# Handing the experts' last rows from ScalarE to VectorE and SyncE, and splitting the last quarter of the output weight in later tiles

## The reference

```python
# 1: q, k, v (2, 8, 768, 64), state (64 x 64) for each head
for t in range(S):
    state = gamma * state + k[t] v[t]^T
    y[t] = scale * q[t] state
# 2: x (1536, 512), 8 experts, w1 (8, 512, 1024), w2 (8, 1024, 512), capacity 384
e = argmax(x @ w_gate); gate = softmax(x @ w_gate)[e]
out[i] = gate * (relu(x[i] @ w1[e]) @ w2[e])      # the first 384 tokens of each expert
# 3: x (1536, 512), w_in (512, 2048), w_out (2048, 512)
h = x @ w_in
P = a0 + a1*h + a2*h^2 + a3*h^3
Q = 1 + |b0|*|h| + |b1|*h^2
out = (P / (Q + 1e-6)) @ w_out
```

## Time and profile before

| | |
|---|---|
| runs | 549.85 us median of 3 (548.81 to 549.91) |
| the profiled execution | 548.83 us, span of the trace 547.0 us |
| granted TensorE clock | 1.00 in all of stage 3 |
| busy, share of the span | TensorE 98%, VectorE 74%, ScalarE 59%, GpSimd 13% |
| stage 2 ends, TensorE's first matmul of stage 3 | 274.2 us |

### The profile page before, as it was taken

The page is one execution under the profiler, slowest core; times in us unless marked ns, Lnnn a source line. Parts: engine busy times, 40 slices in busy tenths (PEclk is TensorE's granted clock), DMA queues, the critical chain, the costliest instruction groups (busy, mean ns, idle before and its releaser), DMA issues.

```text
span 547.0 us, 8985 instructions
## 1 busy us (share of the span) xinstructions
PE 536.8 (98%) x3405; PEld 461.6 (84%) x3405; DVE 404.5 (74%) x737; ACT 320.8 (59%) x484; POOL 73.4 (13%) x71
## 2 busy tenths in 40 slices
PE   8999999999999999999989999999999999999997
PEld 6888889898998989999877878888888888888885
DVE  4567777654747447474869999988888888888885
ACT  3555634554735456465868866657666756665652
POOL 3333314501101011003010001003100000300000
PEclk9999999999999999999999999999999999999999
DMA  9999939959985484922160000001101000100002
GB/s 194 236 253 243 267 111 380 316 192 346 383 346 205 179 286 145 370 120 85 47 218 2 0 20 19 2 1 59 58 1 38 2 1 1 77 1 0 2 1 77
DMA packets 65039, 72.27 MB, mean 132 GB/s; under 512 B 41186, under 2 KB 41698, under 8 KB 64996
## 3 DMA queue, kind: packets, MB, share of 16 engines
q1 hardware_dynamic: 59124, 57.82, 34.2%
q0 software_dynamic: 3136, 9.46, 5.2%
q10 hardware_dynamic: 2736, 4.42, 2.2%
HBM read 59.09 MB, written 12.60 MB: 131 GB/s over the span
## 4 chain that ended last, share of the span: by engine, by line
PE 86%; DVE 4%; ACT 3%; issue 2%; DMA 2%; SPq 1%; ACTq 0%; DVEq 0%
PE bank L848 24%; PE bank L850 24%; PE bank L849 24%; DMA kin<-in_k_dram 2%; PE bank L304 2%; PE bank L270 2%; PE bank L293 1%; SPq L1512 1%; PE bank L812 1%; PE bank L338 1%; PE bank L252 1%; PE bank L284 1%; PE bank L1135 1%; PE bank L259 1%; PE bank L240 1%
## 5 line engine op out<-in xcount | busy, mean ns | idle before, releaser
L782 DVE TENSOR_TENSOR T<-raw,T 128x1024 fp32r<-128x1024 f32 x60 | 71.5, 1222 | 54.7 <-ACT T L776 53.7
L848 PE MATMUL bank<-T,gL 128*128 128x512 f32 x192 | 75.1, 391 | 2.8 <-DVE gL L1382 2.8
L848 PE MATMUL bank<-x2H,T 128*128 128x512 f32 x192 | 75.6, 394 | 0.0
L850 PE MATMUL bank<-x2H,T 128*128 128x512 f32 x192 | 74.8, 389 | 0.0
L849 PE MATMUL bank<-x2L,T 128*128 128x512 f32 x192 | 74.8, 389 | 0.0
L849 PE MATMUL bank<-T,gH 128*128 128x512 f32 x192 | 74.8, 389 | 0.0
L850 PE MATMUL bank<-T,gH 128*128 128x512 f32 x192 | 74.7, 389 | 0.0
L848 PE MATMUL bank<-xH,T 128*128 128x256 f32 x256 | 72.5, 283 | 0.0
L849 PE MATMUL bank<-xL,T 128*128 128x256 f32 x256 | 72.4, 283 | 0.0
L850 PE MATMUL bank<-xH,T 128*128 128x256 f32 x256 | 72.4, 283 | 0.0
L1320 ACT ACTIVATE sq<-bank 128x512 f32<-128x512 f32 x48 | 28.5, 594 | 65.8 <-PE bank L850 65.6
(11 more groups left out here) (156 smaller groups left out, 1040.9 us busy)
## 6 DMA issues: line engine op xcount, KB each, us to landing
raw<-in_moe_w_dram SPq DMA_DIRECT2D x14, 2048.0 KB, 11.1
raw<-in_moe_w_dram SPq DMA_DIRECT2D x8, 512.0 KB, 5.1
ybuf<-ysb ACTq DMA_DIRECT2D x16, 256.0 KB, 5.9
w_out_raw<-in_moe_w_out_dram SPq DMA_DIRECT2D x4, 1024.0 KB, 16.7
qin<-in_q_dram SPq DMA_DIRECT2D x12, 256.0 KB, 5.1
kin<-in_k_dram SPq DMA_DIRECT2D x12, 256.0 KB, 5.7
vin<-in_v_dram SPq DMA_DIRECT2D x12, 256.0 KB, 5.7
xbuf<-xt SPq DMA_DIRECT2D x12, 256.0 KB, 4.2
```

Source lines behind the costliest of these rows:

```text
L782: e.tensor_tensor(W[w][:, 1, cols], raws[par][:, w, cols], W[w][:, 0, cols].bitcast(F32), ALU.subtract).then_inc(r.wL[w], 1)
L848: nc.tensor.matmul(out_, aL, bH, start=start, stop=False)
L850: return nc.tensor.matmul(out_, aH, bH, start=False, stop=stop)
```

## The change

Four things are moved.

- The last rows: the second `act_y` goes. VectorE copies them (`dve_last_y`, behind `dve_win_ready(ready, 1)` and ahead of `dve_wout_ready(ready, 2)`), and SyncE stores them (`sp_last_y`, ahead of its `spilled`).
- `act_wout_late` moves from ahead of tile 0 into tile 7, behind its reciprocal.
- Its two VectorE halves stood ahead of tile 0 and in tile 13; they are in tiles 13 and 15 now.
- Tile 2 on VectorE uses the serial order that only tile 1 had.

```diff
+        def dve_last_y():
+            e = nc.vector
+            s = NMAIN - 1
+            e.wait_ge(main.yst, 16 * (NMAIN * E - 1))
+            e.wait_ge(main.mm2, NMAIN * E)
+            e.tensor_copy(ysb[:, s, :], bank[YB + s][:, :]).then_inc(main.ys, 1)
+
+        def sp_last_y():
+            e = nc.sync
+            s = NMAIN - 1
+            e.wait_ge(main.ys, NMAIN * E)
+            a = 1 + (E - 1) * SLOTS + s * P
+            e.dma_start(ybuf[a:a + P, :], ysb[:, s, :]).then_inc(main.yst, 16)
...
@@ act_last_expert
             act_y(r, i, par, 0)
             act_wout_ready(ready, 2)
-            act_y(r, i, par, 1)
@@ dve_last_expert
             dve_win_ready(ready, 1)
+            dve_last_y()
             dve_wout_ready(ready, 2)
@@ act_block
             elif n == 5:
                 act_win_late(3)
+            elif n == 7:
+                act_wout_late()
@@ dve_block
-            if n == 1:
-                dve_gH(0)
-                dve_back(0)
-                dve_rest(0)
-                dve_gL(0)
-                dve_m(1)
-                dve_cubic(1)
-                dve_linear(1)
+            if n in (1, 2):
+                dve_gH(n - 1)
+                dve_back(n - 1)
+                dve_rest(n - 1)
+                dve_gL(n - 1)
+                dve_m(n)
+                dve_cubic(n)
+                dve_linear(n)
                 return
...
-            elif n == 13:
-                dve_wout_late(1)
+            elif n in (13, 15):
+                dve_wout_late((n - 13) // 2)
@@ sync
-            spilled(e, crowded(e), body, redo)
+            n = crowded(e)
+            sp_last_y()
+            spilled(e, n, body, redo)
@@ scalar
             spilled(e, n, lambda: act_experts(spill), redo)
-            act_wout_late()
             blocks(act_block)
@@ vector
             spilled(e, n, lambda: dve_experts(spill), redo)
-            dve_wout_late(0)
             blocks(dve_block)
```

## The result

The changed kernel takes 546.42 us, median of 5 runs (546.32 to 546.65). The kernel before, in 5 runs, takes 548.90 (548.81 to 549.91); the median of 549.85 shown at first was of three runs, two of them at the upper end. The ratio is 0.995, with an interval of 0.9935 to 0.9964: 2.5 us faster. The profiled execution took 546.42, with a span of 544.6.

What follows compares the result with a forecast made beforehand. TensorE, busy for 98% of the span, was taken as the bound. `dve_linear(7)` comes 3.06 - 0.69 = 2.37 us earlier, the end 2.4: 546.5 from the profiled 548.83, 547.5 forecast from the median 549.85; range 546.0 to 549.4.

Steps and rivals of the forecast that it cites:

- The bound: TensorE's second network: `pe_x2` waits for `dve_linear(7)`, so removing 2.8 us of `gL` waits gains only what `dve_linear(7)` moves.
- Part 1: ScalarE drops the last rows' activation and store: its branch comes at 272.6, ready at 275.5 to 276.5.
- the two bounds: Price of the gap behind ScalarE's branch: 2.87 us by its own rows, 3.86 by the longest record, TensorE's.
- Part 2: Moving `act_wout_late` and its VectorE halves saves 1.82 us on ScalarE, 1.14 on VectorE ahead of tile 0.
- Part 3: VectorE copies the last rows out of PSUM in 0.69 us; behind its branch it is ready at 277.4 to 279.0.
- In time: VectorE is ready for tile 0 by 278.45, its branch's price hidden under its wait for ScalarE.
- not hidden: Rival: VectorE's branch is exposed ahead of tile 0; gain 0.5, time 549.3, or 550.3 at price 3.86; chance 0.14.
- Part 4: SyncE's store of the last rows takes 2.5 us, landing at 277.75, 0.5 to spare before `pa(0)`.
- Part 5: Tile 2 on VectorE in tile 1's order: `gL(1)` comes earlier, at a cost of 0.69 us.

## Why the prediction was right

**The bound.** That the gain is what `dve_linear(7)` moves, and not what the waits for `gL` amount to, held: 2.43 us earlier, 2.5 us gained. Removing the waits for `gL` brought TensorE 3.4 us earlier to the transposes, and 1.0 of this was waited there again; the wait of 1.48 is at the upper end of the 0.9 to 1.5 forecast, for the reason given with it. With the last rows on ScalarE `dve_linear(7)` starts at 316.94, 1.31 earlier than before, and the gain is 1.14. The mixed order of tile 2 and the finer wait of the transposes each moved the time by 0.7 through this place.

**Part 1.** ScalarE's branch moved to 272.6 as said, and its price is 2.8 by the experiment with the split ahead, of the two bounds the lower. `sq(0)` at 277.15 for a forecast of 277.25. That the sequencer runs past a working engine is now shown on ScalarE too: its branch stands at 272.6, beside the operation of 1.92 us that started at 272.56. The Trainium skill, "Runtime: NRT & Kernel Launch", section "Instruction fetch mechanics", says that a taken branch waits for a DMA of its target's page where that page isn't one of the two held. The skips agree: 1.7 or less for a near target, 2.8 for the far one, and for VectorE 0.9 or less against about 4. That the time goes into fetching pages is the page's statement; these runs show that it goes with the length of the skipped code.

**Part 2.** The sum was right and its split was not. I booked 1.82 us on ScalarE and 1.14 on VectorE for the moved split. The run with the split ahead shows 0.07, which is no measurable difference, since the handoff alone makes room for it. Without the handoff the other two parts are worth 1.14 (548.85 to 547.71). So the two are no terms to be added: either takes the gap and the other has what is left up to 277.2, where TensorE sets the start. In tile 7 the copy cost what was said: `dve_m(8)` waited 0.53 us, and TensorE did not notice. The count for tiles 13 and 15 was wrong: four groups of 12 matmuls lie between the end of `pe_in(13)` and `pe_out(12)`, 11.4 us in the trace (342.67 to 354.04), not five and 14. It was enough, as the half of tile 13 ended at 349.7.

**Part 3.** The copy took 0.69, `dve_wout_ready(2)` ended at 277.38, `dve_m(0)` started at 278.37. "In time" was right, but the price of VectorE's branch, bounded at 2.87 to 3.86, is 0.9 or less at this distance. The rival "not hidden" therefore had less to stand on than I gave it: even exposed it cost nothing.

**Part 4.** The landing was mis-sized: 2.8 us for 2.5, so that 0.2 us was to spare, not 0.5. It isn't a fixed figure: in the run with VectorE's branch late the same store, issued at 275.30, took 2.4. The store sits closer to the path than any other step of the change, and from there on each us costs one. The loads of `w_in_late` started at 277.98, not 278.5 to 279.5, and their reader came at 294.03.

**Part 5.** 0.69 priced, 0.70 in the trace, 0.76 in the time without it. Its purpose, to end the wait for `gL(1)`, was hardly needed: 0.2 of it is left in the mixed order.

**The number.** 546.5 was the forecast from the profiled execution of 548.83, and 546.42 was measured. The 547.5 on record came from a median of three runs that lay 0.95 above the later one of five; the difference forecast was 2.4, the measured one 2.5. The range was built on the same median, which is why 546.42 lies near its lower end of 546.0.

## What to carry to other kernels

A stall that one removes is worth only what the next meeting of the same two engines moves: find that place and read how busy the waiting engine's partner is up to there. Two edits that fill or free the same gap don't add, so price them together against what sets the end of the gap. An instruction that makes the sequencer wait (a DMA issue behind an activation, here) should not stand directly ahead of a long jump; and a price seen on one engine's branch says little on another's.

## What was not expected of the hardware

The same branch over unused code costs 0.9 us or less, 2.8 or about 4, by how much code it skips: VectorE 0.9 or less, and about 4 with 300 operations more to jump over; ScalarE 2.8 to 2.9, and 1.7 or less with the skipped body left out. On TensorE its record lasts 3.3 to 3.9 us in all these runs and no wait behind it is listed; in the kernel before matmuls went on beside it until 274.02. A store of 256 KB, with no load of weights beside it, took between 2.0 and 2.8 us to land, and 2.8 or 2.4 at the same place in two kernels. Why VectorE's jump was cheap and ScalarE's was not is open: the lengths of the code that the two skip were not compared, and where each engine's held code ends was not varied.
